# Moving one prefix scan, one transpose and three weight loads in a three-stage attention and expert kernel

## The reference

```python
for t in range(S):                                   # B=4, H=8, S=768, D=48
    cur = einsum('bhd,bhe->bhde', u[None] * k_t, v_t)
    y[:, :, t] = einsum('bhd,bhde->bhe', r_t, state + cur)
    state = w_t[:, :, :, None] * state + einsum('bhd,bhe->bhde', k_t, v_t)
h = x @ w_in                                         # x = y as 3072 x 384, d_ff 2048
x = (h * clip(h + 3, 0, 6) / 6) @ w_out
logits = x @ phi                                     # 8 experts, 4 slots each
d = softmax(logits over tokens); slot_input = d.T @ x
slot_out[e] = relu(slot_input[e] @ w1[e]) @ w2[e]    # width 1024
out = softmax(logits over slots) @ slot_out
```

## Time and profile before

| | |
|---|---|
| median of 3 executions | 422.05 us (421.91 to 425.78) |
| the profiled execution | 421.91 us |
| its span, first to last instruction | 420.2 us |
| PE busy | 402.2 us, 96% |
| DVE busy | 338.0 us, 80% |
| POOL busy | 187.7 us, 45% |
| ACT busy | 162.3 us, 39% |
| mean granted clock of PE | 0.992 |
| HBM read | 64.00 MB |

### The profile page before, as it was taken

One profiled execution on the slowest core, in us unless ns is written; L12 is line 12 of the kernel. 1 busy time (PEld: TensorE's weight loads), 2 busy tenths in 40 slices (PEclk: granted clock), 3 DMA queues, 4 the chain that ended last, 5 costly groups with the idle time before them and its releaser, 6 DMA issues.

```text
span 420.2 us, 9784 instructions
## 1 busy us (share of the span) xinstructions
PE 402.2 (96%) x3914; PEld 220.2 (52%) x3914; DVE 338.0 (80%) x559; ACT 162.3 (39%) x297; POOL 187.7 (45%) x178
## 2 busy tenths in 40 slices
PE   8999999999999999999999999989999999999981
PEld 3884555555555555555555555445553444543430
DVE  7998799998998988989989988989875787661151
ACT  3586256534334244244343333341433234421141
POOL 4445988874555654455744557454540012010000
PEclk9999999999999999999999999999999999999996
DMA  8998331368034213304340331231007099879929
GB/s 245 354 400 277 123 96 29 123 264 274 11 122 122 80 48 123 116 9 123 124 123 2 123 120 51 77 123 58 0 4 297 4 367 411 247 272 420 386 97 357
DMA packets 16397, 69.35 MB, mean 165 GB/s; under 512 B 2144, under 2 KB 2912, under 8 KB 14688
## 3 DMA queue, kind: packets, MB, share of 16 engines
q1 hardware_dynamic: 16352, 68.73, 46.5%
HBM read 64.00 MB, written 4.72 MB: 164 GB/s over the span
## 4 chain that ended last, share of the span: by engine, by line
issue 35%; PE 29%; POOL 22%; DMA 5%; DVE 4%; ACT 1%; POOLq 0%; SPq 0%; DVEq 0%
POOL att L1532 5%; PE hid L568 4%; PE hid L570 4%; DMA att<-rkT_dram 4%; PE hid L569 4%; POOL att L1494 4%; POOL att L1496 4%; POOL att L1517 3%; POOL att L1550 3%; POOL w_split L1508 3%; PE hid L834 3%; PE l_ps L675 2%; PE hid L815 1%; PE sc_ps L815 1%; PE l_ps L615 1%
## 5 line engine op out<-in xcount | busy, mean ns | idle before, releaser
L1343 ACT ACTIVATE relu<-hid,three 128x512 f32<-128x512 f32 x95 | 65.2, 686 | 138.0 <-PE hid L570 137.7
L568 PE MATMUL hid<-x_split,w_split 128*128 128x512 f16 x285 | 108.3, 380 | 0.4 <-DVE gated L997 0.4
L570 PE MATMUL hid<-x_split,w_split 128*128 128x512 f16 x285 | 108.0, 379 | 0.0
L569 PE MATMUL hid<-x_split,w_split 128*128 128x512 f16 x285 | 108.0, 379 | 0.0
L997 DVE SCALAR_TENSOR_TENSOR gated<-relu,hid 128x512 f32<-128x512 f32 x95 | 64.4, 678 | 22.8 <-ACT relu L1343 22.1
L1018 DVE STREAM_TRANSPOSE ring<-gated 128x512 f32<-128x512 f32 x96 | 68.3, 711 | 3.3
L1523 POOL TENSOR_TENSOR att<-att 128x1024 f16<-128x1024 f32 x20 | 40.9, 2045 | 48.4 <-ACT att L1278 48.4
L1541 POOL TENSOR_TENSOR att<-att 112x512 f32<-112x512 f32 x19 | 23.2, 1220 | 57.0 <-DVE att L916 57.0
L568 PEld LDWEIGHTS hid<-x_split,w_split 128*128 128x128 f16 x285 | 27.7, 97 | 36.8 <-DVE gated L997 6.3
L570 PEld LDWEIGHTS hid<-x_split,w_split 128*128 128x128 f16 x285 | 27.8, 98 | 33.7
L569 PEld LDWEIGHTS hid<-x_split,w_split 128*128 128x128 f16 x285 | 27.9, 98 | 25.0 <-issue 0.3
(11 more groups left out here) (269 smaller groups left out, 757.7 us busy)
## 6 DMA issues: line engine op xcount, KB each, us to landing
att<-nat_dram SPq DMA_DIRECT2D x20, 576.0 KB, 4.0
att<-rkT_dram SPq DMA_DIRECT2D x22, 448.0 KB, 5.5
att<-wT_dram SPq DMA_DIRECT2D x22, 226.2 KB, 4.7
att<-w_dram SPq DMA_DIRECT2D x3, 1536.0 KB, 10.0
out_dram<-w_split SPq DMA_DIRECT2D x12, 384.0 KB, 3.9
att<-w_dram SPq DMA_DIRECT2D x5, 768.0 KB, 9.9
stage<-w_in_dram SPq DMA_DIRECT2D x2, 1536.0 KB, 13.6
ring<-w_outT_dram SPq DMA_DIRECT2D x1, 3072.0 KB, 15.2
```

Of the source, the lines that this page charges most:

```text
L568: pe.matmul(hid[s % 2][:], high, x_high, start=(q == 0), stop=False)
L569: pe.matmul(hid[s % 2][:], high, x_low, start=False, stop=False)
L570: last = pe.matmul(hid[s % 2][:], low, x_high, start=False, stop=(q == KT - 1))
L1343: nc.scalar.activation(relu_tile(s), hid[s % 2][:], ACT.Relu, bias=three[:], scale=GATE / H_SCALE)\
```

## The change

Four places are edited; nothing that is computed changes. On SP the wait for the fifth group's gather (`dg_ready`) moves behind the loads of w1 for experts 2 to 4, so that these follow the load of w_out at once. On DVE `scan_prefix` of unit 5 moves from ahead of step 0 into its phase 3, where those of all later units are, `low_v` of unit 4 takes its place, and `low_w(1)` goes ahead of `sum_diag(4)`. On POOL `decay_receptance` of unit 5 goes behind `diag_values` of unit 4. On DVE the transpose `turn_gated(81)`, which stood behind the maximum of the fifth group in step 82, goes to the place that it has in all other groups, behind `gate(81)`.

```diff
             sp.dma_start(att[:, 0:2 * UNIT], w_out).then_inc(w_out_in, 16)
-            sp.wait_ge(dg_ready, 16 * (C - 1))
             for e in range(2, 5):
                 sp.dma_start(w1_place[e], w1[e]).then_inc(w1_in[e // 4], 16)
+            sp.wait_ge(dg_ready, 16 * (C - 1))
             for a in range(2):
                 sp.dma_start(early[a], w2[EARLY][:, a * UNIT // 2:(a + 1) * UNIT // 2]).then_inc(w2_early_in, 16)
...
             mask_first(B)
-            scan_prefix(B + 1)
+            low_v(B)
 
             for s in range(END):
...
                 if s <= 1:
                     gate(s)
-                    if s == 0:
-                        low_v(B)
                     turn_gated(s)
...
                     if 1 <= g < C and i == 2:
-                        if g == C - 1:
-                            turn_gated(s - 1)
                         turn_weight(g - 1)
                         turn_logits(g - 1)
...
                 if s == 0:
+                    low_w(1)
                     sum_diag(B)
-                    low_w(1)
                 if phase == 3:
-                    if is_unit(n + 1) and n > B:
+                    if is_unit(n + 1):
                         scan_prefix(n + 1)
...
-                if 1 < s < STEPS - 2 and s != STEPS - FT + 1:
+                if 1 < s < STEPS - 2:
                     turn_gated(s)
...
             low_scores(B)
-            decay_receptance(B + 1)
             diag_values(B)
...
                 if phase == 3:
-                    if n + 1 < UNITS and n > B:
+                    if n + 1 < UNITS:
                         decay_receptance(n + 1)
```

## The result

| | before | changed |
|---|---|---|
| median | 422.09 us (421.91 to 425.78, 20 executions) | 425.07 us (424.67 to 429.3, 20 executions) |
| ratio to before, 95% interval | | 1.0072 (1.0057 to 1.0085) |
| span of the profiled execution | 420.2 us | 423.3 us |
| PE busy | 402.2 us | 402.6 us |

The change costs 3.0 us. The forecast was 423.4 us, with a range up to 424.9: the direction was right, the size half of what came, and the range missed it. A later batch of experiments ran the changed kernel again: 424.96 us in the median, against 422.24 us for the kernel before in that batch, ratio 1.0053 (1.0030 to 1.0077). The first profiled execution of the changed kernel was an uncommonly long one, 428.6 us, so the readings here are from one of that later batch, 424.99 us, unless they say otherwise.

The account below looks back on a forecast made before the run. The prediction took PE, full and in fixed order, to bound the kernel. Its terms +0.8, +0.7 and 0 made +1.5 us on 421.91 us, forecasting 423.4 us, range 421.8 to 424.9 us.

Parts of the forecast that it names:

- What bounds the kernel: Steps, 100 to 150 us: PE is full, 49.89 of 50 us, in fixed order, so its delays are not made good.
- Edit 1: Start of the steps, reordered DVE and POOL: attend(4) 0.6 us earlier, but score(5) waits for receptances, +0.8 us.
- Edit 2: Step 82, transpose turn_gated(81) ahead of the fifth group's maximum: delays PE's gather, +0.7 us.
- Edit 3: SP's w1 loads for experts 2 to 4 issued some 19 us earlier: nothing waits for them, they cost nothing, 0.
- the fourth rival: PE's 1.4 us idle lowers its clock: 427.3 us, chance 0.04; or earlier loads disturb the instruction stream, same side, 0.02.
- The first two: Rivals: DVE and POOL slow each other only little, 422.0 us, chance 0.10; such a start plus free transpose, 421.3, 0.05.
- The third: Rival: DVE and POOL exclusion hits again in units 5 to 7, up to 0.4 us each: 424.6 us, chance 0.13.

Follow-up runs that it names:

- w_out behind the wait: Kernel before with all three w1 loads ahead of the gather wait and the w_out load moved behind it; 422.14 us against 422.1, ratio 1.0005.
- edit 3 alone: Kernel before with only the w1 loads for experts 2 to 4 moved ahead of the gather wait; 423.95 us against 422.15, ratio 1.0042.
- seventh: Kernel before with low_v(4) first on DVE and unit 5's scan between turn_gated(0) and sum_diag, POOL unchanged; 422.45 us against 422.1, ratio 1.0013.
- eleventh kernel: The seventh kernel's start, plus POOL's low_w(3) one step later, against the kernel before; 423.85 us against 422.24, ratio 1.0032.
- the eighth kernel: Kernel before with only the DVE reordering of Edit 1, POOL's order unchanged; 422.3 us against 422.1, ratio 1.0013.
- tenth: Kernel before with the transpose moved behind the maximum in the fourth group too; 422.61 us against 422.24, ratio 1.0026.
- twelfth: Kernel before with the diffs of the tenth and eleventh kernel together; 423.41 us against 422.24, ratio 1.0018.

## Why the prediction was half right

**What bounds the kernel** held. PE's order is fixed and what it loses it doesn't regain: the shifts at the three places stay to the end and add up to the span's 3.1 us.

**Edit 1, +0.8 forecast, +0.4 measured.** The mechanism held and the size was off. `attend(4)` came at 41.70 against the forecast 41.75; `diag_values` and scan met in the order foreseen. The mis-sized term is POOL's series up to the receptances: it ended at 45.48 where I had 45.85. I had charged an instruction that waits for the other engine with its full duration behind that engine's end, and it takes less. L1492 ended 0.87 behind `low_v(4)` (39.35 less 38.48) where I had 1.0, and `diag_values` 0.62 behind the scan (44.34 less 43.72) where I had 0.82. With some hundredths of overlap at the other changes of instruction that makes the 0.4. The rows of the kernel before had it: there L1496 ended 0.80 behind the scan (39.92 less 39.12), and for `low_v` I did take 0.45 instead of 0.55. The exclusion itself, for which the prediction cites the Trainium skill ("SBUF — State Buffer"), shows again: `low_v(4)` takes 1.32 beside L1490, which ends at 38.06, and 0.42 of it lie behind that end, about the 0.45 that the prediction gave it. Measured are +0.43 in the trace of the changed kernel, +0.51 in that of the edit alone, and +0.4 in the medians, inside the bounds.

**Edit 2, +0.7 forecast, +0.8 measured** in the medians (0.5 in the trace of the edit alone, 0.86 in that of the change), right in each step: maximum, idle of `turn_weight` gone from 0.21 to 0.82, gather's idle from 0.41 to 1.13, and the gather 5.11 us behind `gate(81)` instead of 4.40, which is the 0.7.

**Edit 3, 0 forecast, +1.8 measured. This is the step that failed.** I asked whether anything waits for the loads' data, and rightly found nothing. Then I asked whether they cost, and took the earlier trace rows for the answer: "between 336 and 352 us, with the transfer engines 0.95 busy, PE has 16.00 of 16 us in flight". That shows that PE's reading isn't slowed by full DMA engines. It doesn't show what becomes of a packet of PE's instructions that is due inside a full queue, and the packets at 332.2 and 336.2 came before, and just as, that burst began. The line for "q8 instruction" stood on the page of the kernel before as on this one, and the mechanism was named, as the last words of the fourth rival, with 0.02; its time was never worked out. What could have been read from the trace: w_out (3.1 MB) and three loads are 7.9 MB, at the 382 GB/s of the earlier trace rows 20.7 us, so from 317.12 the engines would be full until 337.8, over the packet of 332.2. If it came only at the end of that, it would be 2.3 us later than 335.50, the start of step 84. Bounds of 0 to 2.3 for this term put the upper end of the range at 423.4 + 2.3 = 425.7 and hold the result, in part by luck: that PE resumes 2.3 to 2.5 us behind the packet, which only the runs showed, isn't in it, and the packet came before the end of the burst.

What the runs showed in its place, by the size of the burst in front of the packet:

| kernel | burst from 317 us | packet at | behind the gather | PE goes on at | cost of the loads |
|---|---|---|---|---|---|
| before | 3.1 MB | 332.2 | 1.0 us | 335.50, no idle | |
| w_out behind the wait | 4.7 MB | 332.2 | 1.0 us | no idle | 0.0 us |
| two loads early (long execution) | 6.3 MB | 337.8 | 2.2 us | no idle | 0.65 us, unlocated |
| edit 3 alone | 7.9 MB | 335.4 | 3.8 us | 337.71 | 1.8 us |
| the change | 7.9 MB | 336.1 | 3.7 us | 338.56 | 1.8 us |

In the last two rows PE resumes 2.3 and 2.5 us behind the packet. Before, it had the packet 3.3 us ahead of need, so there was about 1.0 us to spare: a packet 2.76 us late (335.43 less 332.16 and the 0.51 of the run) costs some 1.7, and that is what edit 3 alone cost in its trace (2.21 less 0.51), 1.8 in the medians. The traces hold two more checks. In the kernels with edits 1 or 2 but the loads as before the packet comes 0.8 to 1.1 us behind the gather. And the next packet, which the kernel before takes at 336.2, 0.7 us behind the start of step 84, comes 4.1 us behind it with edit 3 alone and 4.3 with the change (341.8 and 342.9), as the burst of the two halves of w2 runs out; PE didn't idle there, so that delay cost nothing.

That the full queue delays the packet is shown, by two kernels with it and two without, with the two loads in between. It doesn't wait for the end of the burst: it began some 1.5 us ahead of that in the change (336.1 against 337.5) and just at it with two loads. Why a packet of 16 KB waits 2.6 to 2.8 us for its start, and how the wait grows with a longer burst, stays open; no kernel tried one.

The Trainium skill ("Runtime: NRT & Kernel Launch", on the mechanics of instruction fetch) says that an engine's instructions come in blocks of 16 KB over a DMA queue of its own, ahead of need, and that crossing a block is mostly hidden. The trace agrees on the size (31 packets, 0.51 MB); that it is hidden holds here while the DMA engines have room, and the measured 1.8 us decides against it at step 84 of the kernels whose loads are early.

**The rivals.** The first two are refuted: the receptances were not ready at PE's arrival, and the transpose was not free. The third, a further turn of the exclusion in units 5 to 7, didn't come for the change: `attend(6)` idles 0.54 where it idled 0.48. It did come for the seventh and eleventh kernel, at `attend(5)`. The fourth, a clock that falls after the idle ahead of `score(5)`, didn't come either: PE idled 0.98 there and its matmuls kept their spacing.

## What to carry to other kernels

Before a load is moved earlier, lay its burst (bytes by the rate seen) over the times of the instruction packets that the trace lists, and see whether the queue has room when one is due. An idle of PE with "issue" behind it, where every semaphore that PE waits for has long been given, is the sign to look for a late one. Where DVE and POOL exclude each other, reckon their two-input operations as one queue: a gain in it at one place was paid back ten microseconds later in both kernels that tried it, once with an instruction of POOL that came 0.1 us before one of DVE, once with two of POOL in a row. Here a transpose moved out of an idle gap cost what it takes, and moved within a gapless row it cost nothing.

## What the runs showed beyond this

**The clock fell at idles of 1.77 and 2.81 us.** In the uncommon execution of the changed kernel, 428.6 us, the packet came at 338.1 and PE's idle was longer:

```profile
340.62 0.61 PE L568 MATMUL hid<-x_split,w_split 128*128 128x512 f16 x1 [2.81 <-issue]
341.02 0.63 PE L569 MATMUL hid<-x_split,w_split 128*128 128x512 f16 x1
...
344.14 0.38 PE L568 MATMUL hid<-x_split,w_split 128*128 128x512 f16 x1
344.35 0.38 PE L569 MATMUL hid<-x_split,w_split 128*128 128x512 f16 x1
```

and its stretches:

```profile
340.00:344.00 4.00, 3.38 (x9) 1.26 (x10) 2.09 (x5) 0.00 (x0) 1.83 (x2) 0.57 0.90 360
344.00:348.00 4.00, 4.00 (x31) 1.63 (x30) 2.36 (x4) 1.38 (x2) 0.11 (x1) 1.00 0.00 2
```

Eight matmuls run about 0.42 apart instead of 0.22, at a granted clock of 0.57 on the mean of the stretch, then the clock is back at 1.00; that adds some 1.6 us to the idle. The same fall followed the 1.77 us in the eleventh kernel; behind the 1.70 us of the other execution and the 1.59 of edit 3 alone the granted clock stays at 1.00, its level of 2.4 GHz. In these two cases the lower clock added 1.6 to 1.7 us to the idle. The idle alone doesn't decide: an idle of 1.78 us ahead of `increment(4)` in the trace of the eighth kernel was followed by no fall until another of 1.99 us had come behind it.

**Single executions of most kernels, the one before too, are 4 to 5 us longer** (425.78 in its first three). In the trace of such a one, of the kernel with DVE as in edit 1 and POOL as before, the reason stands at the start: a row of unit 5's decay factors had not landed, where the kernel before has this scan at 34.58 without a wait.

```profile
38.77 1.24 DVE L904 TENSOR_TENSOR_SCAN att<-att 112x517 f32<-112x517 f32 x1 [3.33 <-DMA att<-wT_dram]
```

That trace is 5.5 us above the kernel's median. The wait is 3.33 of them, and most of the rest is the clock: PE then idled 1.99 us ahead of `attend(4)`, and the granted clock is 0.63 on the mean from 48 to 52 us, where it is 1.00 in the kernel before. The long executions of the kernel with two loads early, of the tenth and of the twelfth show the same, a wait of 0.78 to 1.77 us for that row, an idle of 2.3 to 3.4 us ahead of `attend(4)` and a fall of the clock. The long one of the changed kernel does not: it waited 0.20 us for that row, and its fall is the one at step 84. Such executions are fewer than half of each kernel's, so they move the medians little; what delays the row in some and not in others was not tried.
